# The borders between blocks of a fused attention and two-MLP kernel: transposes, banks and queue orders rearranged

## The reference

```python
attn = softmax(rotate(q) @ rotate(k).T / 8)            # 8 heads of 64
x = (attn @ v)                                          # 4 x 576 x 512
xn = (x - mean) / sqrt(var + 1e-6) * g_ln
x = x + relu(xn @ w_ch1) @ w_ch2                        # first MLP, hidden width 2048
u, v = split(gelu(x @ w_in))                            # second MLP
out = x + (u * (w_sg @ layer_norm(v) + b_sg)) @ w_out
```

## Time and profile before

| | us |
|---|---|
| three runs | 942.79, 944.61, 945.11 (median 944.61) |
| profiled execution | 943.27, its span 941.5 |
| TensorE busy | 911.8 (97%) |
| VectorE, ScalarE, GpSimd busy | 703.5, 544.4, 550.2 |

### The profile page before, as it was taken

The page is one execution under the profiler, slowest core; times in us unless marked ns, Lnnn a source line. Parts: engine busy times, 40 slices in busy tenths (PEclk is TensorE's granted clock), DMA queues, the critical chain, the costliest instruction groups (busy, mean ns, idle before and its releaser), DMA issues.

```text
span 941.5 us, 18184 instructions
## 1 busy us (share of the span) xinstructions
PE 911.8 (97%) x6153; PEld 839.8 (89%) x6153; DVE 703.5 (75%) x1155; ACT 544.4 (58%) x1184; POOL 550.2 (58%) x547
## 2 busy tenths in 40 slices
PE   4999999999999999999999999999999999999998
PEld 3899999999989899898889888888888999989897
DVE  4899999999998888843667788779987662663623
ACT  3899999999988566534555555565564321302111
POOL 4989989989863567575566586758875310010100
PEclk9999999999999999999999999999999999999999
DMA  6243243233223233000000000002210001010011
GB/s 176 64 103 93 65 102 91 64 102 91 67 55 94 83 110 102 23 1 1 1 1 1 1 1 1 1 2 68 82 33 2 1 1 45 1 45 12 1 46 56
DMA packets 44873, 44.46 MB, mean 47 GB/s; under 512 B 14016, under 2 KB 34752, under 8 KB 44672
## 3 DMA queue, kind: packets, MB, share of 16 engines
q1 hardware_dynamic: 44368, 43.21, 16.8%
q10 hardware_dynamic: 432, 0.30, 0.1%
HBM read 28.81 MB, written 4.72 MB: 36 GB/s over the span
## 4 chain that ended last, share of the span: by engine, by line
PE 85%; DVE 8%; ACT 3%; issue 2%; POOL 1%; DMA 1%; SPq 0%; ACTq 0%; DVEq 0%; POOLq 0%
PE fc_ps L2130 18%; PE seven_ps L2158 13%; PE ring_ps L2029 8%; PE scores_ps L1965 6%; PE wide_ps L2327 6%; PE wide_ps L2306 5%; PE bank_ps L2283 5%; PE ring_ps L1976 5%; PE bank_ps L2341 5%; PE seven_ps L2210 2%; PE scores_ps L1958 2%; PE ring_ps L1912 2%; DVE hid_sums L1626 2%; PE seven_ps L2130 1%; DVE lefts L1638 1%
## 5 line engine op out<-in xcount | busy, mean ns | idle before, releaser
L2130 PE MATMUL fc_ps<-xT,W1s 128*128 128x512 f32 (+1 forms) x876 | 202.3, 380 | 2.1 <-ACT hid L1142 1.3
L2130 PEld LDWEIGHTS fc_ps<-xT,W1s 128*128 128x128 f32 x876 | 154.0, 189 | 32.3 <-ACT hid L1142 3.1
L2158 PE MATMUL seven_ps<-rights,lefts 128*128 128x256 f32 x1344 | 175.1, 284 | 1.0 <-DVE lefts L1638 1.0
L2158 PEld LDWEIGHTS seven_ps<-rights,lefts 128*128 128x128 f32 x1344 | 170.3, 191 | 5.8 <-DVE lefts L1638 1.2
L942 POOL TENSOR_TENSOR rights<-w_rest,rights 128x256 fp32r<-128x256 f32 x84 | 80.6, 961 | 65.7 <-ACT rights L1185 65.7
L1452 DVE TENSOR_REDUCE nmax<-scores_ps 128x1 f32<-128x576 f32 x144 | 106.7, 752 | 16.0 <-PE scores_ps L1965 11.1
L1048 ACT ACTIVATE E<-scores_ps,nmax 128x576 f32<-128x576 f32 x128 | 95.6, 748 | 11.9 <-DVE nmax L1452 11.1
L1003 POOL TENSOR_TENSOR rstd<-ve,power 128x1 f32<-128x1 f32 x18 | 14.6, 810 | 141.2 <-DVE ve L1822 141.2
L1461 DVE TENSOR_TENSOR prob_lo<-ring_ps,prob_hi 128x512 fp32r<-128x512 f32 x144 | 95.3, 681 | 2.2 <-ACT prob_hi L1062 1.7
L1062 ACT ACTIVATE prob_hi<-ring_ps 128x512 fp32r<-128x512 f32 x144 | 85.5, 612 | 4.3 <-PE ring_ps L1976 2.8
L1142 ACT ACTIVATE hid<-fc_ps 128x512 f32<-128x512 f32 x64 | 37.9, 592 | 80.4 <-PE fc_ps L2130 80.3
(11 more groups left out here) (184 smaller groups left out, 2090.2 us busy)
## 6 DMA issues: line engine op xcount, KB each, us to landing
swapped_k<-stack SPq DMA_DIRECT2D x64, 144.0 KB, 2.5
w_raw<-in_w SPq DMA_DIRECT2D x18, 256.0 KB, 3.1
qk_raw<-in_k SPq DMA_DIRECT2D x16, 256.0 KB, 2.7
v_raw<-in_v SPq DMA_DIRECT2D x16, 256.0 KB, 2.8
qk_raw<-in_q SPq DMA_DIRECT2D x15, 256.0 KB, 2.8
w_rest<-in_w SPq DMA_DIRECT2D x7, 512.0 KB, 4.1
out<-out_sb SPq DMA_DIRECT2D x14, 256.0 KB, 2.4
w_raw<-in_win SPq DMA_DIRECT2D x4, 512.0 KB, 3.6
```

The source lines that it names most:

```text
L2130: mm = nc.tensor.matmul(fc1_bank(n, f)[:, 0:cols], W1s[:, slot1(f), w, c, :], xT[:, x, c, 0:cols], start=first, stop=(c == DC - 1 and x == 1))
L2158: mm = nc.tensor.matmul(seven_ps[k][:, 2 * P * a:2 * P * (a + 1)], lefts[:, k, x, P * a:P * (a + 1)], rights[:, k, w, :], start=(g == 0 an ...
```

## The change

On PE: chunks 2 and 3 of the next block's input move one product later and two products later, so that three products stand between any two chunks. The next block's first two hidden columns stand behind all products of the block; the second one goes into the bank `seven_ps[0]`, which the folds have freed. In the tails block the odd hidden columns (not the even ones from 2) use that bank, and the last tail product is ahead of block 2's hidden columns. In the second MLP's first five value tiles the banks are turned by one (`value_bank`), the tails' chunk is transposed behind all products and is needed only by the last tile, and spatial chunks 3 and 4 are both ahead of that tile.

On ACT and DVE: the last two chunks of a block's successor stand among the folds (`block_end`), all folds of a square stand ahead of its successor's sums, the right operands of a block's first group are made ahead of its first ReLU, and at the start of block 0 `merge_tails((2, 3))` and `right_low_sums` stand behind `left_low` part 2. POOL's code is unchanged.

```diff
...
-SPATIAL = ((), (0, 1), (2,), (3,), (4,))
+SPATIAL = ((), (0, 1), (2,), (3, 4), ())
 def jobs_tv(b):
...
+def value_bank(b, t):
+    return bank_ps[(t + 1) % NT if b == 0 else t % NT]
 def block_pairs(n):
...
 def fc1_bank(n, f):
-    if is_tails(n) and f >= 2 and f % 2 == 0:
+    if is_tails(n) and f % 2 == 1 or n > 1 and f == 1:
         return seven_ps[0]
...
                 act.wait_ge(left_lo, 5 * (at - 1) + 3)
-        nc.scalar.activation(hid[:, f, 0:cols], fc1_ps[:, 0:cols], ACT.Relu).then_inc(hid_relu, 1)
+        nc.scalar.activation(hid[:, f, 0:cols], fc1_bank(n, 2 * g + f)[:, 0:cols], ACT.Relu).then_inc(hid_relu, 1)
     def wait_product(n, g, k):
...
     def right_high_beside(n, g, part):
-        if n > 0 or g > 0:
+        if g > 0:
             right_high(n, g, part)
     def factors(n, g):
-        first, last = place(n) >= 2 and g == 0, g == NG - 1
-        if first:
-            copy_fold(n - 1, 0)
-            next_high(n - 1, 3)
-        if n == 0 and g == 0:
+        first, last = n > 0 and g == 0, g == NG - 1
+        if place(n) >= 2 and first:
+            block_end(n - 1)
+        if first or n == 0 and g == 0:
             for part in range(5):
-                right_high(0, 0, part)
+                right_high(n, g, part)
         relu(n, g, 0)
...
             relu(n, g, 1)
+            next_high(n, 0)
         left_high(n, g, 1)
         right_high_beside(n, g, 1)
-        if last:
-            next_high(n, 0)
         right_high_beside(n, g, 2)
-        if first:
-            copy_fold(n - 1, 1)
         if not last:
...
         right_high_beside(n, g, 4)
-        if last:
-            next_high(n, 2)
+    def block_end(n):
+        copy_fold(n, 0)
+        next_high(n, 2)
+        next_high(n, 3)
+        copy_fold(n, 1)
     def tail_high(f):
...
     def tails_high():
-        copy_fold(0, 0)
-        next_high(0, 3)
+        block_end(0)
+        for f in range(3):
+            tail_w_high(f)
         tail_high(0)
-        tail_w_high(0)
-        copy_fold(0, 1)
         tail_high(1)
-        tail_w_high(1)
-        tail_w_high(2)
         for f in range(2, NF):
...
                 tails_high()
-        copy_fold(NBLK - 1, 0)
-        next_high(NBLK - 1, 3)
+        block_end(NBLK - 1)
         next_high(NBLK - 1, 4)
-        copy_fold(NBLK - 1, 1)
     def mlp2_weights_high(g):
...
                 act.wait_ge(vhat_lo, n - 2)
-            nc.scalar.activation(v_act[:, n % 3, :], bank_ps[t % NT][:, :], ACT.Gelu_apprx_tanh).then_inc(v_gelu, 1)
+            nc.scalar.activation(v_act[:, n % 3, :], value_bank(b, t)[:, :], ACT.Gelu_apprx_tanh).then_inc(v_gelu, 1)
             if b == 0:
...
     def factors(n, g):
-        first, last = place(n) >= 2 and g == 0, g == NG - 1
-        if first:
-            fold(n - 1, 0)
-            next_low(n - 1, 3)
-            for step in range(1, 5):
+        last = g == NG - 1
+        if place(n) >= 2 and g == 0:
+            block_end(n - 1)
+            for step in range(3, FOLDS):
                 fold(n - 1, step)
+        if n > 0 and g == 0:
+            right_low_sums(n, g)
         if n == 0 and g == 0:
...
                 fold_tails(t)
-        if first:
-            fold(n - 1, 5)
-            fold(n - 1, 6)
-        if n == 0 and g == 0:
-            merge_tails((2, 3))
-            right_low_sums(0, 0)
         hid_sum(n, g, S1)
...
         if last:
+            next_low(n, 0)
             left_low(n, g, 1)
-            next_low(n, 0)
         left_low(n, g, 2)
+        if n == 0 and g == 0:
+            merge_tails((2, 3))
+            right_low_sums(0, 0)
         if n == 0 and 0 < g and 2 * g + 3 < NF:
...
             next_low(n, 1)
-        if n > 0 or g > 0:
+        if g > 0:
             right_low_sums(n, g)
         left_low(n, g, 4)
-        if first:
-            fold(n - 1, 7)
-        if last:
-            next_low(n, 2)
+    def block_end(n):
+        fold(n, 0)
+        next_low(n, 2)
+        fold(n, 1)
+        fold(n, 2)
+        next_low(n, 3)
     def tails_low():
-        fold(0, 0)
-        next_low(0, 3)
-        for step in range(1, 5):
+        block_end(0)
+        for step in range(3, 6):
             fold(0, step)
         tail_low(0)
-        fold(0, 5)
         fold(0, 6)
...
                 tails_low()
-        fold(NBLK - 1, 0)
-        next_low(NBLK - 1, 3)
-        for step in range(1, 4):
-            fold(NBLK - 1, step)
+        block_end(NBLK - 1)
+        fold(NBLK - 1, 3)
         next_low(NBLK - 1, 4)
...
             wait_bank_done(3)
-        elif is_tails(n) and f == 2:
-            pe.wait_ge(folded, FREE_FOLDS[0])
-        elif is_tails(n) and f > 0:
-            pe.wait_ge(tail_hid_lo, max(f - 1, 1))
+        elif f == 1 and n > 0:
+            if n == 2:
+                pe.wait_ge(tail_hid_lo, NF)
+            else:
+                pe.wait_ge(folded, FOLDS * (place(n - 1) if n > 1 else 0) + FREE_FOLDS[0])
+        elif is_tails(n) and f > 1:
+            pe.wait_ge(tail_hid_lo, f - 1)
         elif n == 2 and f == 0:
-            pe.wait_ge(tail_hid_lo, NF)
+            pe.wait_ge(tail_hid_lo, NF - 1)
         elif f > 0:
-            pe.wait_ge(hid_relu, place(n) * NF + f)
+            pe.wait_ge(hid_relu, place(n) * NF + (1 if f == 2 and n > 0 else f))
         first = True
...
             if k == 0:
-                pe.wait_ge(tail_hid_lo, NF - 1)
+                pe.wait_ge(hid_relu, place(n) * NF + 2)
             elif k < 3:
...
                 pe.wait_ge(xT_lo, n * DC + k - 2)
+        elif g == 0 and n > 2 and k == 0:
+            pe.wait_ge(hid_relu, place(n) * NF + 2)
         elif g == 0 and n > 2:
...
         if g == NG - 2:
-            steps = [("fc1", 0), 0, ("fc1", 1), 1, ("x", 0), 2, 3, 4, ("x", 1), 5, 6, ("x", 2)]
-        elif g == NG - 1 and is_last(n):
-            steps = [0, 1, ("x", 3), 2, 3, ("tails", 0), 4, 5, 6]
+            steps = [("fc1", 0), 0, ("fc1", 1), 1, ("x", 0), 2, 3, 4, ("x", 1), 5, 6]
         elif g == NG - 1:
-            steps = [0, 1, ("x", 3), 2, 3, ("fc1", 0), 4, 5, ("fc1", 1), 6]
+            steps = [0, ("x", 2), 1, 2, 3, ("x", 3), 4, 5, 6] + ([("tails", 0)] if is_last(n) else [("fc1", 0), ("fc1", 1)])
         m, h = after(n, g)
...
         tail_product(NF - 2)
+        tail_product(NF - 1)
         hidden(2, 0)
-        tail_product(NF - 1)
         hidden(2, 1)
...
     def v_tiles(b):
-        pe.wait_ge(yT_hi, jobs_tv(b + 1))
-        pe.wait_ge(yT_lo, jobs_tv(b + 1))
+        pe.wait_ge(yT_hi, jobs_tv(b + 1) if b > 0 else DC)
+        pe.wait_ge(yT_lo, jobs_tv(b + 1) if b > 0 else DC)
         for t in range(NT + 1 - b % 2):
...
                 pe.wait_ge(v_gelu, jobs_tv(b) + 1)
-            elif b == 0 and t > 0:
-                pe.wait_ge(folded, FOLDS * place(NBLK - 1) + FREE_FOLDS[t - 1])
+            elif b == 0 and t < 3:
+                pe.wait_ge(folded, FOLDS * place(NBLK - 1) + FREE_FOLDS[t])
+            elif b == 0:
+                pe.wait_ge(yT_lo, jobs_tv(1))
             first = True
...
                     lhs = yT[:, a, c, P * t:P * t + P] if t < NT else yTt[:, a, c, :]
-                    mm = nc.tensor.matmul(bank_ps[t % NT][:, :], lhs, winS[:, c, w, DM:2 * DM],
+                    mm = nc.tensor.matmul(value_bank(b, t)[:, :], lhs, winS[:, c, w, DM:2 * DM],
                                           start=first, stop=(c == DC - 1 and w == 1))
...
```

## The result

The changed kernel takes 940.6 us (median of 6 runs, 939.82 to 942.47), the kernel before beside it 943.75: a ratio of 0.9969, 95% interval 0.9956 to 0.9982. That is 3.2 us less, where 4.7 were forecast. Both intervals lie under 1, so the gain is real, but its size differs between the series.

What follows compares the result with a forecast made beforehand. TensorE, 97% busy at full clock, bounds the kernel, so only its gaps count. 1.1 + 1.4 + 1.5 + 1.8 - 1.0 - 0.1 = 4.7 us off 944.0 gives 939.3; range 934.0 to 943.3.

Steps and rivals of the forecast that it cites:

- Part 1: Borders 2/3 and 3/4: input transposes x0 to x3 three products apart hide their chain, except 0.4 us lost at x3.
- Part 2: Same borders: three hidden columns in a row, 8.25 us, no wait for folded; 1.48 us won up to here.
- Part 3: Blocks 3 and 4: TensorE waits 2.6 us (0 to 2.6) before product 2, VectorE going one for one with GpSimd.
- rival (a): Start of blocks 3 and 4: no collision of VectorE and GpSimd; 9.5 us won in all, 934.5; chance 0.24.
- Rival (c): Start of blocks 2 to 4: GpSimd holds VectorE out for whole instructions; 1.4 us slower, 945.4; chance 0.10.
- -1.0 and -0.1: Blocks 3 and 4 together, with their borders and the new wait: 1.1 us slower.
- 1.35 us of old waits: Block 4 behind its border: waits in the old trace, 1.1 us of them expected gone (0 to 1.35).
- Parts 4 to 7: Border 0 to tails wins 1.4 us, tails to block 2 1.5, start of block 0 1.1, border to MLP2 1.8.
- (b): Rival: copy_fold and fold 0 ahead of chunk 2 cost 0.8 us more at four borders; 1.5 won, 942.5; chance 0.16.

Runs made afterwards that it cites:

- e4: The changed kernel with the next block's chunk 2 served ahead of copy_fold(0) on ScalarE and fold 0 on VectorE: 938.35 us.
- e6: The changed kernel with GpSimd's additions in groups 1 to 4 and chunk 2 served ahead of copy_fold(0) and fold 0: 931.78 us.
- e1: The changed kernel with GpSimd's four additions to Y of blocks 2 and 3 moved from the new block's first group to groups 1 to 4: 933.71 us.
- e2: The changed kernel with each GpSimd addition to Y written as two instructions of half the width at the same place: 934.59 us.
- e8: The second series: the changed kernel itself run again, nothing edited, eleven runs: 941.74 us, the kernel before 943.25, ratio 0.9981.
- e7: The kernel of e1, with TensorE's third product in blocks 3 and 4 also waiting for two unneeded low parts of the next group: 939.34 us.

## Why the prediction was right

**Part 1** (spacing) held. Between x1 and x2 are 2.69, x0 and x1 2.61; the fourth waits 0.49, and x2 to x3 are 3.27, 0.60 more than the 2.67 of e4, which has no wait (0.40 forecast). What was short: VectorE's left_low(4) ahead of it took 1.22 beside a right_low of GpSimd's, and fold 0 behind it gave way to the split only at 529.08, where the reckoning, moved to this clock by 4.38, had 528.67. At border 0/tails there is no wait (2.37 apart) where 0.34 was forecast: the chunks are half as wide.

**Part 2** held as written: three hidden columns from 532.58 to 540.76, 8.18, no wait for `folded`. e4 and e6 confirm that the order in which the fourth chunk is served made the wait that was left.

**Part 3**, the step with the doubt, came out at 2.47 us of idle (542.19, when the two products had ended, to 544.66) for 2.6 forecast, in both blocks. The path came out step by step: the reckoning had left_low(2) ready for TensorE at 548.7, and 544.66 is 548.70 when moved by the 4.04 between 544.80 and 540.76. e1 shows that GpSimd's additions are the cause, e2 that it is one for one by instruction. So rival (a) fell; its price was about right, though: e1, where the collision is taken away, is 9.9 below the kernel before, for the 9.5 of (a). Rival (c), whole instructions and no overlap, falls too: 1.43 to 1.54 apart, not 1.70.

**What was mis-sized** is the pair of terms -1.0 and -0.1 for blocks 3 and 4. From the first transpose to hidden columns 4 of block 3 are 29.68, for 28.29 before (525.78 to 554.07): 1.4 lost where 1.0 was reckoned. The 0.4 more is there already when hidden columns 0 start (11.18 behind the first transpose, 10.77 reckoned). In block 4 the 1.35 us of old waits were all gone (28.35 from 635.37 to 663.72, less 1.68, is 26.67, for 26.66 of work; 1.1 forecast), but the half clock took 1.68 in this execution. The prediction priced the idle time as idle and left out what it does to the clock behind it. The table's 2.7 against its 4.8 is this 1.7 and 0.4 of small misses. 4.7 - 1.7 = 3.0 stands beside the 3.2 measured. With both waits followed by it, it would be 4.7 - 2 x 1.7 = 1.3, beside the 1.5 of the second series; but by the estimate at e8 only four of those eleven runs had two, so the smaller gain of that series isn't fully explained. Its 941.74 lies inside the forecast range and on the far side of the 941.5 that the prediction had set as the border of "faster": the direction holds in both series, the size only in the first.

**Parts 4 to 7**: 1.66 for 1.4, 1.62 for 1.5, 1.17 for 1.1. At the border to MLP2, the last transpose waits 0.33 and the first value tile comes 0.77 earlier than the shift brought so far (1.0 forecast; the shift is 1.17 at the first transpose, 1.94 at the tile); with the u chunk's wait gone it makes 1.56 of the 1.8.

**Rivals.** (b) named a real cost but not its size: the fourth chunk's service costs 0.60, 0.60 and about 0.4, all of which e4 and e6 get back (1.7 by their profiled executions), while (b) had put 0.8 on top of the reckoned 0.4 at four borders. That its 1.5 is also the gain of the second series doesn't speak for it: the profile of that series has the same waits as the first.

## What to carry to other kernels

When work is packed more tightly ahead of a deadline, look at what runs beside it: here each VectorE instruction with two SBUF inputs let one GpSimd instruction go first, so put GpSimd's long instructions where VectorE has slack, or cut them. And a wait of 2 to 3 us on TensorE can cost more than its length, since the matmuls behind it may run at half clock; behind the waits of under 1 us in the MLP of the kernel before, no 20 us stretch had a clock under 1.00. Serve a chain that TensorE waits for ahead of bookkeeping of the same engines.

## What the runs showed of the hardware that was not expected

- TensorE's clock fell to 0.50 (1.2 GHz) after 2.30 to 2.88 us of idle, in a program that keeps TensorE 97% busy. It fell behind some such waits and not behind others of the same length (2.30 in both blocks of the changed kernel, 2.31 in both of e4), and not behind 1.62 in e7. Each time it cost 1.56 to 1.68 us, half to three quarters of the wait again.
- What decides between two equal waits isn't shown: in the changed kernel the fall came in the block with 0.2 us more of idle behind the wait (both profiles), in e4 in the one without.
- The row of the granted clock doesn't show everything. At the start of every program it reads 1.00, yet in the changed kernel matmuls of 288 columns stand 0.24 apart there (14.98 to 15.22) and 0.13 later (24.54 to 24.67); the change of pace comes at about 23 us in the kernel before, 24 in the changed one and 25.5 in e1. Distances between equal matmuls are the surer sign.
- Six half-width additions on GpSimd took 5.58 us beside VectorE, three whole ones 4.34, and the kernel with the halves was 6 us faster.
- Fold steps, which read PSUM and one SBUF operand, took 0.67 to 0.69 each in all kernels, whatever GpSimd did beside them.
